# Stage 0 of a delta-rule attention and two-MLP kernel in an order of its own on six PSUM banks, and new step tables for all stages

## What is computed

```
# attention: a 48x48 state per batch and head
for t in range(768):
    y[t]  = q[t] @ state
    state = state + beta[t] * outer(kn[t], v[t] - kn[t] @ state)   # kn = k / |k|
x = y as 3072 tokens x 384
# first MLP, 384 -> 2048 -> 384
h = max(x @ w_in, 0);  x = (h * h) @ w_out
# second MLP, 384 -> 1536 -> 384
y = (sigmoid(x @ w_gate) * (x @ w_val)) @ w_out2
```

## Time and profile before

| | us |
|---|---|
| median of 3 runs | 1008.27 (1006.84 to 1010.36) |
| profiled execution | 1009.32 |
| its span | 1007.50 |
| first matmul of the first MLP | 95.13 |
| first matmul of the second MLP | 583.97 |
| TensorE busy | 960.3 (95%) |
| VectorE busy | 543.4 (54%) |
| ScalarE busy | 481.4 (48%) |

### The profile page before, as it was taken

How to read it: one execution, slowest core, us unless ns; L and a number is a source line. 1 busy time by engine, 2 the same in 40 slices (tenths; PEclk the granted TensorE clock), 3 DMA queues, 4 the chain that set the end, 5 groups by cost and what they waited for, 6 DMA issues and landing times.

```text
span 1007.5 us, 23481 instructions
## 1 busy us (share of the span) xinstructions
PE 960.3 (95%) x10030; PEld 491.6 (49%) x10030; DVE 543.4 (54%) x1075; ACT 481.4 (48%) x865; POOL 13.2 (1%) x27
## 2 busy tenths in 40 slices
PE   2876999999999999999999999999999999999998
PEld 1464565465456456546544444444444444444443
DVE  6978957957866885794326542432422422423322
ACT  4874575666576477556659832132222222222221
POOL 0000000000000000000000000000000000000000
PEclk7867999999999999999999999999999999999999
DMA  9515015015004202201124010010100100100000
GB/s 310 122 35 127 2 34 126 35 35 127 32 4 97 62 34 62 67 33 36 62 92 159 1 63 1 0 62 0 41 21 0 62 0 0 62 0 0 31 0 31
DMA packets 20996, 52.16 MB, mean 52 GB/s; under 512 B 2672, under 2 KB 12912, under 8 KB 20528
## 3 DMA queue, kind: packets, MB, share of 16 engines
q1 hardware_dynamic: 20320, 50.60, 17.8%
q10 hardware_dynamic: 592, 0.33, 0.2%
HBM read 41.48 MB, written 9.44 MB: 51 GB/s over the span
## 4 chain that ended last, share of the span: by engine, by line
PE 88%; DVE 5%; issue 2%; ACT 2%; DMA 1%; SPq 0%; POOL 0%; DVEq 0%; POOLq 0%
PE psum L642 75%; PE psum L556 3%; PE psum L487 1%; PE psum L513 1%; DMA raw_a<-in_w_in 1%; PE psum L543 1%; PE psum L500 1%; PE psum L571 1%; PE psum L525 1%; ACT w L825 1%; PE psum L585 1%; DVE work L1130 1%; PE psum L452 1%; DVE attn L1089 1%; ACT w L731 1%
## 5 line engine op out<-in xcount | busy, mean ns | idle before, releaser
L642 PE MATMUL psum<-work,attn 128*128 128x512 f16 x1944 | 419.9, 379 | 0.1
L642 PE MATMUL psum<-work,w 128*128 128x512 f16 x1728 | 386.3, 380 | 9.7 <-issue 5.9
L642 PEld LDWEIGHTS psum<-work,attn 128*128 128x128 f16 x1944 | 190.2, 98 | 229.7 <-DVE work L1130 0.6
L642 PEld LDWEIGHTS psum<-work,w 128*128 128x128 f16 x1728 | 164.3, 98 | 204.5 <-issue 9.5
L731 ACT ACTIVATE work<-work 128x512 f16<-128x512 f32 (+1 forms) x264 | 155.7, 624 | 143.3 <-DVE work L1263 140.2
L1263 DVE SCALAR_TENSOR_TENSOR work<-psum,work 128x512 f32<-128x512 f32 x72 | 49.8, 692 | 273.0 <-PE psum L642 261.8
L731 ACT ACTIVATE work<-psum,scal 128x512 f32<-128x512 f32 x90 | 60.5, 687 | 169.6 <-PE psum L642 169.5
L1111 DVE SCALAR_TENSOR_TENSOR work<-work 128x512 f16<-128x512 f16 x96 | 66.1, 690 | 61.6 <-ACT work L731 59.8
L731 ACT ACTIVATE attn<-psum 64x384 f32<-64x384 f32 (+5 forms) x160 | 66.0, 442 | 66.2 <-PE psum L513 34.6
L731 ACT ACTIVATE work<-psum 128x512 f32<-128x512 f32 x96 | 57.2, 596 | 64.3 <-PE psum L642 62.9
L1069 DVE TENSOR_TENSOR attn<-attn 128x31 f32<-128x31 f32 (+15 forms) x186 | 63.7, 343 | 6.4
(11 more groups left out here) (97 smaller groups left out, 558.7 us busy)
## 6 DMA issues: line engine op xcount, KB each, us to landing
attn<-in_kt SPq DMA_DIRECT2D x24, 192.0 KB, 4.3
attn<-in_v SPq DMA_DIRECT2D x24, 192.0 KB, 4.5
attn<-in_kn SPq DMA_DIRECT2D x24, 192.0 KB, 3.8
x_spill<-work SPq DMA_DIRECT2D x6, 768.0 KB, 3.4
xt<-x_spill SPq DMA_DIRECT2D x6, 768.0 KB, 5.1
attn<-in_qt SPq DMA_DIRECT2D x20, 192.0 KB, 4.2
y_out<-work SPq DMA_DIRECT2D x5, 768.0 KB, 3.6
work<-in_w_out SPq DMA_DIRECT2D x1, 3072.0 KB, 24.3
```

What stands on the lines that cost most here:

```text
L642: m = mm(dst, x, z, start=first and i == 0, stop=last and i == len(a) - 1)
```

## The change

Stages 2 to 5 get other steps. The rows of the columns stand at step 15 instead of 6 (14 instead of 11 in stage 1), and `start` at 23 instead of 15 (25 instead of 18), so that most of a group's columns lie in its own stage. Group 1's columns may use only the steps of stage 0 that lie before its `xsplit`. Stage 0 gets an order of its own with 18 steps up to `xsplit`, six banks (PSUM 5, 6, 7, 2, 3, 4) given by which was filled longest ago, a place for reading a fill that can be later than the fill (`READ_LATER`), the half copies `place_e` in two parts, the 12 pieces of the first low weight in three lots of four with `kk` of group 1 in between, and its warming matmuls behind fills (4, 1, 4, 2 and 14). The largest x is taken for the two chunks apart, and ScalarE makes the high parts of x in stage 0. `split_x` waits for one part of each cutting instead of all; the rest is waited for by the first `hidden_act` and the first `rest_of_hidden`, and the last two small parts and the last low part of the second weight are cut behind `split_x`. The keys of group 1 are loaded right behind the weights. Counts of matmuls and reads of the attention are the same.

```diff
-PLACE = dict(rows=6, scale_v=8, mid=(8, 11), off=(10, 14), qk=(-4, 10), ks=(8, 15), dr=(11, 16), grow=(13, 20), xt=(18, 21), xmax=23, xscale=27, xsplit=31, kk=(3, 5), lanes=14, norm=15, start=15)
+PLACE = dict(rows=15, scale_v=15, mid=(15, 16), off=(16, 22), qk=(-3, 4), ks=(15, 22), dr=(17, 24), grow=(19, 26), xt=(23, 26), xmax=27, xscale=29, xsplit=31, kk=(1, 13), lanes=21, norm=21, start=23)
...
+    0: dict(kk=(0, 1), qk=(2, 9), mid=(3, 5), off=(4, 7), dr=(6, 13), grow=(8, 14), ks=(-7, 10), xt=(11, 15), lanes=3,
+            norm=3, root=7, xmax=16, xscale=17, xsplit=18, start=13, place_e=(3, 8), hi_out=(1, 9, 9, 10), small=(9, 12, 19, 19),
+            first_out=(7, 11, 13, 19), first_max=13),
+    1: dict(rows=14, scale_v=15, mid=(16, 16), off=(17, 21), qk=(1, 5), ks=(17, 23), dr=(20, 24), grow=(22, 26), xt=(25, 27), xmax=29, xscale=31, xsplit=31, kk=(8, 11), lanes=20, norm=23, start=25),
...
+READ_LATER = {("qk", 0, 1, 0): 12, ("qk", 0, 1, 1): 12, ("off", 0, 0, 1): 9}
...
+    _n = NB_FIRST if _s == 0 and (_kind, _g) != ("kk", 1) else NB
+    _b = min(range(_n), key=lambda b: _last[b])
...
-    steps = [(g - 1, step) for step in range(start, STEPS)]
+    steps = [(g - 1, step) for step in range(start, STEPS if g > 1 else place(0, "xsplit"))]
...
-REST_BANK, REST_PIECES = (2, 3, 4, 1, 5, 6, 7, 2, 3, 4, 1, 2), 12
-REST_FIRST = 12
+REST_PIECES = 12
+REST_BANK = (1, 3, 4, 2) * 3
+REST_AT = {OPEN: (0, 1, 2, 3), 0: (4, 5, 6, 7), 1: (8, 9, 10, 11)}
-WARM_AHEAD = ("mid", "off", "qk", "ks", "dr")
+WARM_BEHIND = {("mid", 0, 0): 4, ("mid", 1, 1): 1, ("dr", 1, 1): 4, ("su", 1, 1): 2, ("xt", 1, 1): 14}
...
             def hidden_act(k, m):
                 n = N1 * m + k
+                if n == 0:
+                    act.wait_ge(w_small_done, W_PIECES)
+                    act.wait_ge(w_out_done, W_PIECES)
...
+            def first_high_parts():
+
+                act.wait_ge(x_scaled, 5)
+                act.wait_ge(w_small_done, 1)
+                act.wait_ge(w_out_done, 1)
+                for kc in range(KC):
+                    run(x_hi[:, kc], xt32[:, TOK * kc:TOK * (kc + 1)], scale=cell(X + 2)).then_inc(x_cut, 1)
...
+            def max_of_chunk(c):
+
+                for x in range(2):
+                    wait_taken(dve, "xt", 0, c, x)
+                link(V.tensor_reduce(scal[:, 32 + KC * c:32 + KC * (c + 1)],
+                                     xt32[:].rearrange("p (k c f) -> p k c f", k=KC, c=NC)[:, :, c], AX.X, ALU.max,
+                                     apply_absolute_value=True), xmax_first, c + 1)
```

## The result

The kernel after takes 1010.78 us (median of 20 runs, 1008.74 to 1012.97), the kernel before beside it 1008.94 us (20 runs, 1006.84 to 1010.76). The ratio is 1.0021 (1.0014 to 1.0028): within 0.3%, on the slow side, and 7.2 us above the forecast. The profiled execution took 1011.15 us, its span 1009.4 us.

What follows compares the result with a forecast made beforehand. TensorE, busy from the first hidden product on, was taken as the bound: 10.0 (chain) - 2.3 (clock) - 4.7 (stage 1) + 1.7 (waits) = 4.7 us off 1009.32, with the median 1.05 lower: 1003.6 us, range 1000.5 to 1006.7 (8 in 10: 998.5 to 1008.8).

Steps and rivals of the forecast that it cites:

- stage 0, chain and clock: Stage 0 up to the first hidden product: shorter chain saves 10.0 us, links at 1.2 GHz cost 2.3.
- stage 1, its 0.6 of waits included: Stage 1: VectorE's work up to the first transpose loses 4.7 us; 0.6 of a transpose's wait comes back.
- stages 2 to 5: Columns spread over twelve more steps: 1.1 us of `project` waits for VectorE taken back, the rest costing nothing.
- mid 0.6 (half of L513's 1.20): Stage 0 chain: mid follows qk on TensorE, takes 0.6 us and ends at 51.7.
- takes 1.15 to 56.5: Stage 0 chain: the solve of chunk 0 starts at 55.4 and takes 1.15 us, to 56.5.
- near 88.6: End of stage 0: the first hidden product (L662) should start near 88.6 us in the new profile.
- I take the queries of chunk 1 and ks at 1.2 GHz: Stage 0, behind the longest hole: these two TensorE links run at the low clock, costing 2.3 us.
- The second rival: Stage 0: all later links of chunk 1 also at 1.2 GHz (3.7 us); 1007.3 us, no change; chance 0.22.
- the forecast's own sign (less than 3): Stage 1: the forecast is wrong if its waits come to less than 3 us or more than 6.5.
- The transposes come a step behind the `su` of which they waited: Rest of stage 1, after the mids: transposes placed one step behind `su`; no size of its own given.
- The two waits that I took back: Stages 2 to 5: of three `project` waits for VectorE (2.0 us), 0.9 placed in stage 6, 1.1 taken back.
- the rival of VectorE late by several us a stage: Stages 2 to 5: VectorE pauses 4.8 us per stage, less 1.2 slack, 14.4 in all; 1018.0 us, slower; chance 0.08.

Runs made afterwards that it cites:

- e3: Kernel after with 9, 16 and 24 (instead of 14) warming matmuls in the three holes of TensorE in stage 0; 1009.68 us, ratio to before 1.0008.
- e11: Kernel after without any warming matmuls behind fills (the 11 at the start stay); 1013.85 us, ratio to before 1.0063.
- e6: Kernel after with columns 1 to 10 of group 1 not computed, so its result differs; 1007.81 us, one run.
- e7: Kernel after with group 1 prepared earlier and 13 of its columns in steps 8, 9 and 13 of stage 0; 1007.64 us, ratio to before 0.9990.
- e4: Kernel after with its new stage 0 but before's tables for stages 1 to 5; 1011.7 us, ratio to before 1.0031.
- e9: Kernel of e7 with the warming matmuls of e3 added; 1004.52 us, ratio to before 0.9959.
- e1: Kernel after with the last transposes of stages 2 to 5 at step 27 instead of 26, the maximum at 28; 1009.38 us, ratio to before 1.0006.
- e2: Kernel after with the second mid of stage 1 at step 18 instead of 16; 1010.81 us, ratio to before 1.0018.

## Why the prediction was wrong

The forecast saved 4.7 us of span and 1.8 were lost, a miss of 6.5. By its own terms:

| term | predicted | measured |
|---|---|---|
| stage 0, chain and clock | 10.0 - 2.3 = +7.7 | +3.5 |
| stage 1, its 0.6 of waits included | -4.7 + 0.6 = -4.1 | -4.2 |
| stages 2 to 5 | +1.1 | -1.1 |

Three terms of the sum failed: the chain was 2.6 us too short, the clock cost 4.1 in stage 0 and not 2.3, and stages 2 to 5, priced at a gain, lose 1.1. The term of stage 1 came out right by luck.

**The chain's durations and hand-overs, 2.6 us.** One step that failed is "mid 0.6 (half of L513's 1.20)". A row with x64 was one half already, as after's row at 51.47 shows: 1.20. With that, a start 0.4 us later and a half of `place_e` of 1.27 instead of 1.05, the first solve starts at 56.53 instead of 55.4. The other step is "takes 1.15 to 56.5": the solve took 2.3 us, with a gap of 0.87 us inside it for which the profile shows no releaser, and its reading on ScalarE starts at 58.88 where the forecast has the first copies from 56.5. From there the links have about the lengths I gave them. The queries of chunk 1 are 2.6 us late (66.41 against 63.8); the second solve is 2.0 late (76.92 against 74.9, the 72.6 of the chain and 2.3 for the clock), since the two cold links cost 1.7 and not 2.3; and its own 0.8, which I had not counted, makes the first product 2.6 late (91.24 against 88.6). That banks and order bring the start forward was right; the forecast "near 88.6" wasn't.

**The clock, 1.8 us in stage 0 and 1.7 in stage 1.** "I take the queries of chunk 1 and ks at 1.2 GHz" had the right two links (0.88 + 0.80, against 2.3 forecast). The clock did come back with the second outputs, as forecast: it was up from 80.8 us and they start at 80.64. What was put at nothing is the solve in between (0.8) and a second fall, from 91.1 us on, under the first product, which took 1.59 us more than at full clock, though before's first product was cold too. In all 4.1 us of links in stage 0 and, at 132 us, 1.7 more in stage 1. The second rival ("the gain is eaten at the clock", 1007.3 us) came nearest by its number; of the links it names only the solve was cold, and it has nothing of the first product or of stages 1 to 5. e3 shows that the clock can be held in just these links, e11 what it costs when nothing holds it.

**Stage 1: the sum of VectorE right, the loss it makes half of it.** I laid out 37.6 us from the last low part of x to the first transpose; measured are 37.2 (92.4 to 129.65), and TensorE's own work is 32.2 as predicted. But the two waits are 1.38 + 1.31, not 4.7, because the cold first product gave VectorE 1.6 us and more. By the forecast's own sign (less than 3) that was wrong. All waits of stage 1 together grew by 3.2 (4.4 against 1.2, the 0.78 of a `project` at 182.69 and the 0.39 of `ks` among them), the clock at 132 us added 1.7, and TensorE's own work in the stage is 0.7 shorter: 4.2. The total is right by chance: two sizes off, in opposite directions, and one of them, the fall at 132, came in only two of the twelve executions. That VectorE's ten columns make the waits is shown by e6 (columns out: 87.46), by e7 (columns in the pauses: 87.03) and by e4 (not the table).

**What I priced at nothing.** I took VectorE's load as fixed and asked only where its end falls. That it stood idle for 10.4 us in stage 0 (the earlier trace rows has the pause of 4.11 in the old order) and that the same columns fit there was not weighed; it decides the change. e7 against after: 3.1 us, and with the clock held, e9: 6.3 us.

**Stages 2 to 5.** "The transposes come a step behind the `su` of which they waited" is true of stage 1 alone. In `PLACE` both stand at 26 now (`grow=(19, 26)`, `xt=(23, 26)`), where before they stood at 20 and 21. And the earlier trace rows had the price: the one wait of L585 for L1105, 0.6 us, came from stage 1, whose old table had `grow` and `xt` both at 26. Four stages now pay it, 2.4 us. The two waits that I took back did go, 0.48 us in stage 2 and 0.62 in stage 5; the third, 0.89, lies at the end of stage 5 (517.78 us) and not in stage 6, and stays. As forecast, L520 doesn't wait in these stages, and the rival of VectorE late by several us a stage is refuted; but e1 shows that VectorE has no slack there: with the wait taken away at one place, two thirds of it come at the next.

**What stays open.** What makes the clock fall at 132 us in some executions, and the gap within the first solve. It is there in all eleven traces that have this stage 0, 0.41 to 0.87 us long, and in ten of them behind the same 34 records of the solve. In e11, where five warming matmuls fewer run ahead of it, it comes five records later:

```profile
56.38 0.96 PE L563 MATMUL psum<-attn 64*64 64x48 f32 x39 [0.41 <-ACT attn L750]
57.75 0.98 PE L563 MATMUL psum<-attn 64*64 64x48 f32 x25 [0.41 <-issue]
```

So its place goes by the count of instructions in TensorE's own program, and not by another engine. That points to the loading of instructions (after's trace has a transfer of 16 KB on a queue of the kind "instruction" just before 56 us, ahead of the gap at 57.31), but no run tests it.

## What to carry to other kernels

When an engine with pauses early becomes the bound later, count the pauses before counting its load: moving work from after a hand-over into a pause before it won 3.1 us here (e7), while the shorter chain alone lost 2.7 (e4). Two losses that overlap, here a cold TensorE ahead of an engine that is late, must be mended together: the clock alone won 1.1 us (e3), the pauses alone 3.1 (e7), both 6.3 (e9). And when a table changes, look for pairs of producer and consumer that now share a step: a wait that the trace shows once, in the one stage where they shared it before, is the price in every stage.

## What the runs showed of the hardware

A busy TensorE is no sign of a high clock, nor the reverse. In e9, TensorE busy for 9.16 of 12.0 us had 2.4 GHz, and right behind that, in full use, it had 1.2:

```profile
67.00:79.00 12.00, 9.16 (x219) 1.00 0.53 116
79.00:82.40 3.40, 3.40 (x41) 0.50 0.43 105
```

After's stretch of 67.2 to 80.8 us (9.73 of 13.6 us busy) had 0.50; e9's has 16 matmuls on zeros among the same links. The Trainium skill ("TensorE: Matmul & The Clock Gate", section "What's actually happening") has the clock throttled by default and released by activity. That e3 and e9, with more matmuls in the holes, had 2.4 GHz there and e11, with fewer, fell three times between 56 and 88 us agrees with it; the earlier trace rows (busy 3.41 of 3.41 us at 0.50) and after's stretch do not.

The places where the clock falls aren't fixed. After and e3 have the same instructions there, and from 37.7 to 41.1 us after ran at full clock and e3 at half. Of the eleven traces with this stage 0, six have such a cold stretch near 40 us (e1, e2, e3, e6, e7, e9) and five have not. With it the first queries start at 50.79 to 51.53 us, without it at 49.14 to 49.46. One profiled execution can thus be 1 to 2 us off in stage 0 by this alone, so the small differences of stage 0 between these kernels are read from the medians.
